# The dispatch softmax of a soft mixture of experts, taken in two blocks of tokens

## The reference, cut to what matters

```
def _moe_ref(x, phi, w1, w2):
    logits = x @ phi                         # tokens x 32 slots (8 experts x 4 slots)
    d = logits - logits.max(0, keepdims=True)
    d = np.exp(d)
    d /= d.sum(0, keepdims=True) + 1e-09     # dispatch: softmax over all tokens
    slot_input = d.T @ x                     # 32 slots x 512
    for e in range(E):                       # 4 slots of each of 8 experts
        h = np.maximum(slot_input[e] @ w1[e], 0.0)
        slot_out[e] = h @ w2[e]
    c = logits - logits.max(1, keepdims=True)
    c = np.exp(c)
    c /= c.sum(1, keepdims=True) + 1e-09     # combine: softmax over the slots
    return c @ slot_out
```

## Time and profile before

| | us |
|---|---|
| median of 3 runs | 325.69 (325.08 to 326.36) |
| profiled execution | 325.23, of which the span of instructions is 323.4 |
| PE busy | 310.2 (96% of the span) |
| DVE busy | 207.8 (64%) |
| ACT busy | 138.0 (43%) |
| POOL busy | 64.2 (20%) |
| granted TensorE clock, mean | 0.999 of full speed |

### The profile page before, as it was taken

How to read it: one execution, slowest core, us unless ns; L and a number is a source line. 1 busy time by engine, 2 the same in 40 slices (tenths; PEclk the granted TensorE clock), 3 DMA queues, 4 the chain that set the end, 5 groups by cost and what they waited for, 6 DMA issues and landing times.

```text
span 323.4 us, 7773 instructions
## 1 busy us (share of the span) xinstructions
PE 310.2 (96%) x2968; PEld 220.6 (68%) x2968; DVE 207.8 (64%) x427; ACT 138.0 (43%) x290; POOL 64.2 (20%) x61
## 2 busy tenths in 40 slices
PE   7899999999999998999989999999999999999994
PEld 4577777777777784333432888878888888888883
DVE  4888988988988466411334868476666666666672
ACT  1466656666767441001217654252225222432431
POOL 0533533433434000000002996000000000000000
PEclk9999999999999999999999999999999999999999
DMA  6999999999996895799999500030003000300202
GB/s 219 390 374 357 365 361 421 379 362 409 378 389 234 334 397 208 292 351 428 409 387 387 201 0 2 0 131 2 0 0 130 2 0 0 131 3 0 97 2 73
DMA packets 19664, 69.56 MB, mean 215 GB/s; under 512 B 4016, under 2 KB 5552, under 8 KB 16048
## 3 DMA queue, kind: packets, MB, share of 16 engines
q1 hardware_dynamic: 19632, 69.14, 56.9%
HBM read 64.41 MB, written 4.46 MB: 213 GB/s over the span
## 4 chain that ended last, share of the span: by engine, by line
PE 87%; DVE 6%; issue 5%; ACT 0%; POOL 0%; DVEq 0%; POOLq 0%
PE ps L789 20%; PE ps L792 20%; PE ps L517 5%; PE ps L562 5%; PE ps L766 5%; PE ps L692 4%; PE ps L720 4%; PE ps L554 3%; PE ps L533 3%; DVE sc L1026 3%; PE ps L573 3%; PE ps L508 2%; PE ps L527 2%; PE ps L548 2%; PE ps L625 2%
## 5 line engine op out<-in xcount | busy, mean ns | idle before, releaser
L792 PE MATMUL ps<-wlo,gg 128*128 128x512 f32 x204 | 80.5, 395 | 0.0
L789 PE MATMUL ps<-whi,gg 128*128 128x512 f32 x204 | 80.2, 393 | 0.0
L1182 DVE SCALAR_TENSOR_TENSOR nt<-uu,ps 128x512 f32<-128x512 f32 (+2 forms) x80 | 48.4, 607 | 47.4 <-ACT uu L933 47.1
L933 ACT ACTIVATE uu<-ps 128x512 f32<-128x512 f32 (+2 forms) x80 | 42.7, 536 | 83.3 <-PE ps L766 77.4
L425 POOL TENSOR_TENSOR sc<-sc,mx 128x640 f32<-128x640 f32 x32 | 40.0, 1252 | 53.5 <-DVE mx L1031 53.5
L1193 DVE TENSOR_TENSOR gg<-nt,ps 128x512 fp32r<-128x512 f32 (+2 forms) x80 | 47.9, 601 | 0.1
L789 PEld LDWEIGHTS ps<-whi,gg 128*128 128x128 f32 x204 | 38.4, 188 | 8.8
L792 PEld LDWEIGHTS ps<-wlo,gg 128*128 128x128 f32 x204 | 38.3, 188 | 8.0
L1026 DVE TENSOR_TENSOR sc<-ps,cst 128x640 f32<-128x640 f32 x32 | 26.2, 820 | 7.2 <-DMA cst<-consts 3.0
L766 PE MATMUL ps<-cT,Pst 128*128 128x512 f32 (+2 forms) x80 | 29.2, 369 | 0.0
L562 PEld LDWEIGHTS ps<-vv,eT 128*64 128x64 f32 x512 | 18.7, 136 | 13.4 <-issue 11.1
(11 more groups left out here) (113 smaller groups left out, 376.2 us busy)
## 6 DMA issues: line engine op xcount, KB each, us to landing
w<-moe_w SPq DMA_DIRECT2D x12, 2048.0 KB, 9.9
vv<-v_t SPq DMA_DIRECT2D x8, 1170.0 KB, 7.3
w<-moe_w SPq DMA_DIRECT2D x8, 1024.0 KB, 12.2
kT<-k_t SPq DMA_DIRECT2D x16, 416.0 KB, 5.8
out<-oo SPq DMA_DIRECT2D x17, 256.0 KB, 2.2
qT<-q_t SPq DMA_DIRECT2D x16, 256.0 KB, 6.8
win<-moe_w_in SPq DMA_DIRECT2D x4, 1024.0 KB, 15.8
wout<-moe_w_out SPq DMA_DIRECT2D x4, 1024.0 KB, 14.6
```

Of the source, the lines that this page charges most:

```text
L789: pe.matmul(o, g, hi, start=(c == 0), stop=False)
L792: mm = pe.matmul(o, g, lo, start=False, stop=(c == NC - 1))
L933: nc.scalar.activation(uu[c % 2][:, 0:width], cols(h_bank(i, c), width), ACT.Square, scale=(1.0 / 3) ** 0.5).then_inc(square_ready, 1)
L1182: nc.vector.scalar_tensor_tensor(out=nt[c % 2][:, 0:width], in0=uu[c % 2][:, 0:width], scalar=1.0, in1=cols(h_bank(i, c), width), op0=ALU. ...
```

## The change

The 17 tiles are split into two blocks, tiles 0 to 7 and 8 to 16. Each has its own column maximum, its own reduction on POOL, its own subtraction, exponential and matmuls (into PSUM banks 4 and 0). The two are joined with factors exp(block maximum - overall maximum) per slot: eight small matmuls turn them onto the partitions, ACT scales the first block's result (`front`), and DVE adds the second's. The division by the sum is left out of `slots` and is done in the factor behind the first layer's rectifier (`expert_scale`), which is possible as the factor is positive. Tile 16's logits are computed with tokens on the partitions directly (`last_logits`), without copy and turning back. The combine softmax starts later, behind `slotT`. The two dummies ahead of the slot matmuls go; the one behind them stays, on `w1s[0]`, behind a wait for the first four loads of `w1`. The load of `w2s[3]` waits for the first block (`front_in_ready`) and no longer for all. The logits move by 256 columns in PSUM, so that the first block lies in bank 5 and the second in bank 6.

```diff
@@ SP
             sp.wait_ge(logits_ready, NG)
             load_w1(sp, 7, w1_each_loaded[7], w1s[7][:])
-            sp.wait_ge(slot_in_ready, 1)
+            sp.wait_ge(front_in_ready, 1)
             load_w2(sp, 3, w2_loaded, w2s[3][:])
@@ POOL
-            pool.wait_ge(router_steps, 1)
-            nc.gpsimd.partition_all_reduce(allmax[:], colmax[:], P, RMAX).then_inc(allmax_ready, 1)
+            for b in range(2):
+                pool.wait_ge(colmax_ready, b + 1)
+                nc.gpsimd.partition_all_reduce(blockmax[:, b, :], colmax[:, b, :], P, RMAX).then_inc(blockmax_ready, 1)
@@ PE
+            def last_logits():
+                pe.wait_ge(xT_copied_act, 2 * NG)
+                pe.wait_ge(xT_copied_dve, 2 * NG)
+                for f in range(4):
+                    mm = pe.matmul(logits_of(NT - 1, 1), xT[:, (NG - 1) % 2, f, 0:P], phi_sb[:, f, :],
+                                   start=(f == 0), stop=(f == 3))
+                mm.then_inc(logits_ready, 1)
...
-            turn_logits(NG - 1)
-            stay_awake(2, 7, cst)
-            pe.wait_ge(d_exp_ready, 1)
-            for t in range(NT):
...
-            stay_awake(1, 0, cst)
+            last_logits()
+            turn_logits(NG - 2)
+            def slot_in(block, bank, first, last):
+                pe.wait_ge(d_exp_ready, block + 1)
+                for t in range(first, last):
+                    g = t % 4
+                    mm = pe.matmul(ps[32 * g:32 * g + 32, bank, :], dd[:, t, :], x[:, t, :],
+                                   start=(t < first + 4), stop=(t + 4 >= last))
+                    if block and t == first + 2:
+                        pe.wait_ge(factors_ready, 1)
+                        for b in range(2):
+                            for j in range(4):
+                                own = pe.matmul(ps[32 * j:32 * j + 32, FACTOR_BANK, b:b + 1], factors[:, b, :],
+                                                ident[:, 0:1], start=True, stop=True)
+                        own.then_inc(factors_turned, 1)
+                mm.then_inc((front_in_ready, slot_in_ready)[block], 1)
+            slot_in(0, FRONT_BANK, *BLOCKS[0])
+            slot_in(1, REST_BANK, *BLOCKS[1])
+            pe.wait_ge(w1_loaded, 64)
+            stay_awake(1, 1, w1s[0][:, 0, :])
             pe.wait_ge(slots_ready, 1)
             fold(slots, 7, slotsT_ready)
+            pe.wait_ge(dsum_scaled, 1)
+            for j in range(4):
+                for b in range(2):
+                    one = pe.matmul(ps[32 * j:32 * j + 32, SUM_BANK, 0:1], dsum[:, b, :], cst[:, C_ONE:C_ONE + 1],
+                                    start=(b == 0), stop=(b == 1))
+            one.then_inc(d_sum_ready, 1)
@@ ACT
+            for b, (first, last) in enumerate(BLOCKS):
+                act.wait_ge(d_lowered, b + 1)
+                nc.scalar.activation(dd[:, first:last], dd[:, first:last], ACT.Exp).then_inc(d_exp_ready, 1)
+            act.wait_ge(factors_lowered, 1)
+            nc.scalar.activation(factors[:], factors[:], ACT.Exp).then_inc(factors_ready, 1)
+            act.wait_ge(front_in_ready, 1)
+            act.wait_ge(own_factor_ready, 1)
+            nc.scalar.activation(front[:], cols(FRONT_BANK, 512), ACT.Copy, scale=own_factor[:, 0:1]).then_inc(front_scaled, 1)
+            act.wait_ge(c_lowered, 1)
             nc.scalar.activation(cc[:], cc[:], ACT.Exp).then_inc(c_exp_ready, 1)
...
-                                     scale=cst[:, C_EXP + g:C_EXP + g + 1]).then_inc(hidden_copied_act, 1)
+                                     scale=expert_scale[:, g:g + 1]).then_inc(hidden_copied_act, 1)
@@ DVE: the order of the router's end (each name is a function or one instruction)
+            max_of(0)
+            copy_tokens(NG - 1)
+            lower_d(0)
+            out_logits(NG - 2)
+            max_of(1)
+            lower_d(1)
+            nc.vector.tensor_tensor(allmax[:], blockmax[:, 0, :], blockmax[:, 1, :], ALU.max).then_inc(allmax_ready, 1)
+            nc.vector.tensor_tensor(factors[:], blockmax[:], allmax[:].unsqueeze(1).broadcast_to([P, 2, 32]),
+                                    ALU.subtract).then_inc(factors_lowered, 1)
+            sum_d(0)
+            sum_d(1)
+            nc.vector.tensor_copy(own_factor[:], cols(FACTOR_BANK, 2)).then_inc(own_factor_ready, 1)
+            nc.vector.tensor_tensor(dsum[:], dsum[:], factors[:], ALU.mult).then_inc(dsum_scaled, 1)
+            nc.vector.scalar_tensor_tensor(out=slots[:], in0=cols(REST_BANK, 512), scalar=own_factor[:, 1:2], in1=front[:],
+                                           op0=ALU.mult, op1=ALU.add).then_inc(slots_ready, 1)
```

More of the change, by code:

```diff
@@ L135, in program @@
         rowinv = place("rowinv", [P, NT], F32)
-        colmax = place("colmax", [P, 32], F32)
+        colmax = place("colmax", [P, 2, 32], F32)
+        blockmax = place("blockmax", [P, 2, 32], F32)
         allmax = place("allmax", [P, 32], F32)
-        dsum = place("dsum", [P, 32], F32)
+        factors = place("factors", [P, 2, 32], F32)
+        dsum = place("dsum", [P, 2, 32], F32)
+        own_factor = place("own_factor", [P, 2], F32)
+        expert_scale = place("expert_scale", [P, 2], F32)
         rD = place("rD", [P, 2], F32)
@@ L155, in program @@
         soT = place("soT", [P, 4, 32], F32)
+        front = place("front", [P, DM], F32, mask_at)
         cc4 = [place("cc40", [P, 4, 4, 32], F32, dd_at), place("cc41", [P, 4, 4, 32], F32, mask_at)]
@@ L632, in turn_logits @@
                 pe.wait_ge(logitsT_copied, g + 1)
-                pe.transpose(cols(5, n, P * g), lT[0:n, g % 2, :], cst[0:n, C_ID:C_ID + n]).then_inc(logits_ready, 1)
-            for g in range(NG + 1):
+                pe.transpose(logits_of(4 * g, n // 32), lT[0:n, g % 2, :], cst[0:n, C_ID:C_ID + n]).then_inc(logits_ready, 1)
+            def last_logits():
[5 more added lines that the diff above has]
+                mm.then_inc(logits_ready, 1)
+            for g in range(NG):
                 if g == NG - 1:
@@ L683, in first_layer @@
             def first_layer(g, half):
-                if g == 0 and half == 0:
-                    pe.wait_ge(w1_loaded, 64)
+                if g == 1 and half == 0:
+                    pe.wait_ge(c_lowered, 1)
                 for j in range(4 if g and half == 0 else 0):
@@ L1077, in out_logits, with copy_tokens @@
                 nc.vector.tensor_copy(lT[0:n, g % 2, :], cols(4 + 3 * (g % 2), P)[0:n, :]).then_inc(logitsT_copied, 1)
-            for g in range(NG):
+            def copy_tokens(g):
                 n = P * min(4, NT - 4 * g)
@@ L1103, in _, with max_of @@
-            dve.wait_ge(d_sum_ready, 1)
-            nc.vector.tensor_scalar(rD[:, 0:1], cols(7, 1), EPS, None, ALU.add).then_inc(sums_ready, 1)
-            dve.wait_ge(sums_ready, 1)
-            nc.vector.reciprocal(rD[:, 1:2], rD[:, 0:1]).then_inc(sums_ready, 1)
+            def max_of(b):
+                first, last = BLOCKS[b]
+                dve.wait_ge(logits_ready, (2, NG)[b])
+                by_slot = logits_of(first, last - first).rearrange("p (t s) -> p s t", s=32)
+                nc.vector.tensor_reduce(colmax[:, b, :], by_slot, AX.X, ALU.max).then_inc(colmax_ready, 1)
@@ new lines, in lower_d, with sum_d @@
+            def lower_d(b):
+                first, last = BLOCKS[b]
+                n = last - first
+                dve.wait_ge(blockmax_ready, b + 1)
+                nc.vector.tensor_tensor(dd[:, first:last], logits_of(first, n).rearrange("p (t s) -> p t s", s=32),
+                                        blockmax[:, b, :].unsqueeze(1).broadcast_to([P, n, 32]), ALU.subtract).then_inc(d_lowered, 1)
+            def sum_d(b):
+                first, last = BLOCKS[b]
+                dve.wait_ge(d_exp_ready, b + 1)
+                nc.vector.tensor_reduce(dsum[:, b, :], dd[:, first:last].rearrange("p t s -> p s t"), AX.X, ALU.add).then_inc(dsum_ready, 1)
@@ new lines, in _ @@
+            copy_tokens(0)
+            for g in range(1, NG - 1):
+                copy_tokens(g)
+                out_logits(g - 1)
+            max_of(0)
[5 more added lines that the diff above has]
+            nc.vector.tensor_tensor(allmax[:], blockmax[:, 0, :], blockmax[:, 1, :], ALU.max).then_inc(allmax_ready, 1)
+            dve.wait_ge(allmax_ready, 1)
+            nc.vector.tensor_tensor(factors[:], blockmax[:], allmax[:].unsqueeze(1).broadcast_to([P, 2, 32]),
+                                    ALU.subtract).then_inc(factors_lowered, 1)
```

73 lines of the change are left out of this document (34 added, 39 removed).

## The result

The changed kernel takes 323.84 us (median of 6, 323.24 to 324.63); the kernel before, measured beside it, 326.28 (median of 6). The ratio is 0.9921, with a 95% interval of 0.9897 to 0.9946: faster by 2.4 us, or 0.8%. The profiled execution took 323.24 us, its span 321.3 us for 323.4 before, so 2.1 us of the 2.4 are in the two profiles. Medians and ratios from here on leave out executions that fell in a slower state, over 1.5% above the fastest of their kernel (two of e3, one each of e11 and e12).

What follows compares the result with a forecast made beforehand. PE (87% of the span) bounds the kernel, with the load stream ending together with it behind the router. PE gains 2.67 us, loads let 2.5 through: 325.23 - 2.5 = 322.7 profiled, 323.2 against the median; range 322.1 to 325.0.

Steps and rivals of the forecast that it cites:

- Logits complete: Router's end: without tile 16's copy and turning, all logits are complete at 124.67 us, 0.36 earlier.
- To the second block: From logits to the second block's matmuls: shorter maximum, subtraction and exponential save 0.26, 0.27 and 0.27 us; start at 126.71.
- The slot matmuls: Second block: three rounds, 2.58 us, plus 0.45 for eight one-column matmuls, together 3.03; end at 129.74, 2.67 earlier.
- The join: Joining both blocks: the first block's scaling is over near 129.0, ahead of the slot matmuls' end at 129.74.
- the second rival: At the blocks' joining: it costs a round or DVE is late, gain 1.65 us, time 324.0; chance 0.10.
- From there to the first layer: Slot matmuls' end to first layer: fold and slotT follow at the same distance as before; first layer at 132.1.
- Sum on PE: PE's work up to the first layer: 2.67 us earlier in all.
- The loads: Stream of w2 halves, w_in and w_out: starts 1.8 to 2.7 us earlier, taken as 2.5 of PE's 2.67.
- The first rival: At the load stream: halves start at 137.3 with their slow start behind, gain 1.8 us, time 323.9; chance 0.15.
- The prediction's own sign that it is wrong: At PE's waits for w2: growth by more than 0.5 us, one of three signs named as refuting the forecast.
- The clock: PE's granted clock between 120 and 140 us: not under 1.00, though two dummies of 2 us together are gone.
- the fourth rival: Before the first layer: without dummies the clock falls to 1.2 GHz, 4.7 - 2.5 us, time 327.9; chance 0.06.

Runs made afterwards that it cites:

- e3: The kernel before without its three dummy matmul groups: 328.80 us (7 of 9 runs), ratio 1.0085 to the kernel before.
- e11: The changed kernel with w2's second halves loaded in quarters, PE waiting for the last only mid-part, and w_out's first quarter in four pieces: 322.90 us, ratio 0.9912.
- e12: The changed kernel once more, unaltered, for comparison within the same call: 323.78 us, ratio 0.9930 to the kernel before.
- e5: The changed kernel with w2's first halves loaded in quarters, each issued once its quarter of the first layer is through: 323.91 us, ratio 0.9912.
- e9: The changed kernel with the load of w2s[3] left out, expert 3 reading expert 2's weights: 322.62 us, ratio 0.9892 to the kernel before.
- e8: The changed kernel without its last dummy, the one behind the slot matmuls: 324.09 us, ratio 0.9939 to the kernel before.
- e10: The kernel before with only tile 16's logits computed the new way, without copy and turning: 325.32 us, ratio 0.9975.
- e4: The changed kernel with the load of w2s[3] waiting for all slot matmuls again: 323.86 us, ratio 0.9936; its profiled execution took 326.99 us.

## Why the prediction came out right, step by step

The time (323.84, forecast 323.2, range 322.1 to 325.0) and the sign were right. The gain of 2.4 us agrees with the forecast of 2.5, but that is in part luck: PE gained 0.4 us more than forecast and the loads took 0.8 more, and the two errors ran against each other. By the two profiles the gain is 2.0 us (325.23 to 323.24).

- **Logits complete**: forecast 0.36 earlier, measured 0.66. `last_logits` took 0.81 us and not 1.0, so a good part of the 0.38 of the earlier trace rows was start-up, as suspected; and the turning behind it added 0.15 on the chain, not 0.26, as its start lay beside the last of the matmuls.
- **To the second block**: forecast 0.80, measured 0.78 (from 2.83 to 2.05). The three short operations came out at 0.47, 0.47 and 0.45 us for 0.46, 0.46 and 0.40. The reduction took 0.56 where 0.63 stood.
- **The slot matmuls**: forecast 3.03 us, measured 2.88 (126.43 to 129.31): three rounds and about 0.3 us for the eight one-column matmuls.
- **The join**: `front` was ready at 128.62, 0.7 us before the second block's end, so the second rival did not come to pass. DVE's two sums took 1.17 us for the 1.3 assumed.
- **From there to the first layer**: 2.38 us in both kernels, as said.
- **Sum on PE**: 3.10 us, forecast 2.67.
- **The loads**: this is the term that was mis-sized. I let them take 0.17 us; they took 1.0 (tail 189.6 for 188.6), and 0.6 in e12's profile. I sized it by when the stream of halves starts: "the halves' own slow start [...] will lie beside the end of `w2s[3]`". That step failed. The windows still show the slow start, and e5, which issued the halves earlier, did not remove it. But the slow start is not what the change lost by: the kernel before has one too (172 GB/s at 139 to 140), and the first half's ninth landing stands 8.5 us behind the first layer in both kernels, the last half's at 25.9 and 26.1. So the middle of the stream moved by nearly all of PE's 3.1 us. What PE waits for is the last landing of 16, and that moved by 2.1 only (from 162.1 to 160.1); its lag behind the ninth went from 1.4 to 2.3 us. Why it grew stays open (e9).
- **The first rival** had the right place, and its price (0.9 us off PE's 2.7) was close to what happened, but its reason, a late start of the halves, was not the one. The prediction's own sign that it is wrong, a wait of PE for `w2` grown by more than 0.5 us, did show: 1.48 for 0.45. PE's first matmul on `w_out`'s first piece began at 175.88, forecast 175.4.
- **SP's queue**: the eight issues of halves took 6.22 us where 5.29 stood before (the fourth alone 2.06, the first 0.33). As the last half's ninth landing moved by only 0.2, late issues did not hold the load as a whole; whether they held its slowest engine is not shown.
- **The clock** stayed at 1.00 in the changed kernel, as forecast, but the fourth rival was better founded than its 0.06: e3 shows that the kernel before without its dummies loses 2.4 us by it. In the changed kernel the first block's matmuls stand in for them, as e8 shows against e3.

What is not settled: which DMA engines are late and why, and how much of e9's gain is the rest and how much the 2.1 MB left out. Of PE's 3.1 us only the 0.65 of the last logits was measured by itself (e10); the rest is divided by the timelines.

## What to carry to other kernels

A reduction over all tokens ahead of a matmul leaves TensorE waiting; taking it in blocks with running maxima and joining them by factors gives it real work in the place of dummies, at the price of a few very short instructions. When PE and a stream of loads end together, count both, and count the stream by the landing of its last part on its slowest engine, not by its mean rate; if PE can begin on a first part while the last still lands (e11), that lateness is hidden. Before taking dummies away, look at how long PE would rest where they stood.

## What was not expected of the hardware

- The 16 landings of one half of `w2` spread by 0.7 us (e9's first ones) to 4.8 us (e4's last). For the first load of `w_in` the last landing came 1.5 us after the ninth in the kernel before, 2.3 in the changed one, 4.5 in e4's profiled execution.
- A PE rest of 2.76 us, ended at 162.77, was followed by a mean granted clock of 0.75 in 165 to 170 us (e4). The kernel with a rest of 2.85 us had a lower mean clock in seven of nine executions but not in the other two, one of which is the profiled one (e3).
- On POOL, going from a reduction to ordinary arithmetic cost 6.6 to 11.2 us in these runs, and going back 9.5 us, with nothing visible in between; a second reduction straight behind cost nothing.
